# Windowed attention ahead of two dense layers: value means gathered by one product and spread by GpSimd, keys read where they lie

## What is computed

```python
k_sum = k.reshape(B, H, nb, block, D).max(axis=3)      # block 32, nb = 24
v_sum = v.reshape(B, H, nb, block, D).mean(axis=3)
scores_l = scale * np.matmul(q, k.transpose(0, 1, 3, 2))
mask_l = np.abs(pos[:, None] - pos[None, :]) < window   # window 16
scores_s = scale * np.einsum('bhsd,bhnd->bhsn', q, k_sum) + np.log(block)
scores_l_m = np.where(mask_l, scores_l, -1000000000.0)
a = softmax(np.concatenate([scores_l_m, scores_s], axis=-1))
attn = np.matmul(a, np.concatenate([v, v_sum], axis=2))
...
h = np.maximum(x @ w_in, 0.0);  x = h * h @ w_out       # layer 1
h = x @ w2_in;  out = (P(h) / Q(h)) @ w2_out            # layer 2, P cubic, Q quadratic
```

## Time and profile before

| what | value |
|---|---|
| median of three runs | 617.87 us (617.2, 617.87, 619.64) |
| the profiled execution, its own time | 619.3 us |
| its span in the profile | 617.2 us |
| granted TensorE clock, mean of the span | 0.999 |
| PE busy / DVE / ACT / POOL | 581.2 / 443.0 / 261.6 / 147.2 us |
| instructions | 9768 |

### The profile page before, as it was taken

The page is one execution under the profiler, slowest core; times in us unless marked ns, Lnnn a source line. Parts: engine busy times, 40 slices in busy tenths (PEclk is TensorE's granted clock), DMA queues, the critical chain, the costliest instruction groups (busy, mean ns, idle before and its releaser), DMA issues.

```text
span 617.2 us, 9768 instructions
## 1 busy us (share of the span) xinstructions
PE 581.2 (94%) x3360; PEld 473.0 (77%) x3360; DVE 443.0 (72%) x839; ACT 261.6 (42%) x556; POOL 147.2 (24%) x158
## 2 busy tenths in 40 slices
PE   4587899999999999999999989999999999999995
PEld 3465678888888888888888867788888888888884
DVE  5467798765343333356765699999999999999996
ACT  4477731110131110311110855566766566766564
POOL 6255640000030000120000566622222222222220
PEclk9999999999999999999999999999999999999999
DMA  8477544000000000023322200000100000100001
GB/s 252 100 212 246 191 163 184 0 1 0 1 1 0 0 0 0 0 68 103 103 102 102 69 1 0 1 0 1 68 0 0 0 0 0 69 1 0 1 1 68
DMA packets 13535, 32.55 MB, mean 53 GB/s; under 512 B 1728, under 2 KB 4416, under 8 KB 13504
## 3 DMA queue, kind: packets, MB, share of 16 engines
q1 hardware_dynamic: 13360, 31.99, 16.1%
q10 hardware_dynamic: 144, 0.13, 0.1%
HBM read 27.79 MB, written 3.15 MB: 50 GB/s over the span
## 4 chain that ended last, share of the span: by engine, by line
PE 46%; DVE 35%; issue 9%; ACT 3%; DMA 3%; SPq 2%; DVEq 1%; POOL 0%; POOLq 0%
PE bank L533 22%; PE bank L585 21%; DVE ratio L981 9%; DVE numer L963 6%; DVE ratio L975 5%; DVE numer L961 5%; DVE ratio L970 5%; DVE hhi L988 4%; DMA kraw<-kT 3%; ACT prob L665 2%; SPq L262 1%; PE bank L502 1%; PE bank L519 1%; DVE hlo L992 1%; PE bank L483 1%
## 5 line engine op out<-in xcount | busy, mean ns | idle before, releaser
L533 PE MATMUL bank<-xhi,whi 128*128 (+1 forms) x384 | 149.8, 390 | 0.1
L533 PE MATMUL bank<-xhi,wlo 128*128 (+1 forms) x384 | 149.4, 389 | 0.0
L533 PE MATMUL bank<-xlo,whi 128*128 (+1 forms) x384 | 149.4, 389 | 0.0
L443 POOL TENSOR_TENSOR denom<-denom,habs 128x512 f32<-128x512 f32 (+1 forms) x49 | 62.3, 1273 | 251.0 <-ACT denom L736 251.0
L678 ACT ACTIVATE hsq<-bank 128x512 f32<-128x512 f32 x48 | 28.8, 600 | 213.2 <-PE bank L533 213.1
L533 PEld LDWEIGHTS bank<-xhi,whi 128*128 128x128 f32 x384 | 72.1, 188 | 15.2 <-issue 0.3
L533 PEld LDWEIGHTS bank<-xhi,wlo 128*128 128x128 f32 x384 | 72.1, 188 | 15.1
L533 PEld LDWEIGHTS bank<-xlo,whi 128*128 128x128 f32 x384 | 72.1, 188 | 14.7
L600 PE MATMUL bank<-whi,hhi 128*128 128x512 f32 x192 | 75.9, 395 | 7.6 <-DVE hlo L992 7.6
L600 PE MATMUL bank<-wlo,hhi 128*128 128x512 f32 x192 | 74.8, 390 | 0.0
L600 PE MATMUL bank<-whi,hlo 128*128 128x512 f32 x192 | 74.8, 390 | 0.0
(11 more groups left out here) (69 smaller groups left out, 862.2 us busy)
## 6 DMA issues: line engine op xcount, KB each, us to landing
wraw<-w SPq DMA_DIRECT2D x32, 512.0 KB, 4.1
vwin<-vw SPq DMA_DIRECT2D x16, 288.0 KB, 5.4
q<-qT SPq DMA_DIRECT2D x8, 384.0 KB, 6.0
out<-osb SPq DMA_DIRECT2D x12, 256.0 KB, 2.1
kraw<-kT SPq DMA_DIRECT2D x7, 384.0 KB, 6.1
vwin<-vsum SPq DMA_DIRECT2D x32, 36.0 KB
kraw<-kT SPq DMA_DIRECT2D x2, 128.0 KB, 2.4
kraw<-kT ACTq DMA_DIRECT2D x1, 128.0 KB, 2.7
```

The costliest lines, as they stand in the source:

```text
L443: g.tensor_tensor(denom[:, i, cols], denom[:, i, cols], habs[:, i, cols], ALU.mult).then_inc(q_done, 1)
L533: last = mm(hps[j % 2][:, :], W[a][:, j, kt * P:(kt + 1) * P], X[b][:, kt, bass.ds(CH * c, CH)], start=kt == 0 and i == 0, stop=kt == KT - ...
```

## The change

`kwin` is gone. `scores` reads its 96 local keys from `kraw` in place, in 8 products of 96 columns, and the block maxima from `ksum` in 8 further products of 24 columns into the same PSUM tile. SP's key loads wait for `s_done` in the place of `windows_ready`. The four pieces of value means are copied to `sums` (`copy_sums`), gathered on PE into 24 consecutive rows at partition 96 by one product with a matrix of ones and zeros `pick` (`gather`), copied to `vsum` (`copy_summary`), and copied by POOL behind the local rows of `vwin`, one copy of 24x512 for each group (`spread`). The four transfers of each pair are gone, and SP's loads stand in plain order of pairs. `SUMMARY_AT` puts `summary` of pairs 1 and 2 at groups 1 and 4 (before 1 and 3), and of the later pairs one group later than before.

```diff
@@ -66,7 +66,7 @@
-SUMMARY_AT = [0, 1, 3] + [GPB * n - 4 for n in range(3, NB)]
+SUMMARY_AT = [0] + [GPB * n - 2 - (n > 2) for n in range(1, NB)]
...
 def unit(j, h):
-        kwin.append(places[far](f"kwin{r}", [P, NW, COLS]))
+    sums = places[0]("sums", [P, P])
...
+    pick = area("pick", [P, 32])
...
@@ -236,7 +238,7 @@
         def load_k(n):
             if n >= RING:
-                sp.wait_ge(windows_ready, GPB * (n - RING + 1))
+                sp.wait_ge(s_done, GPB * (n - RING + 1))
             sp.dma_start(kraw[n % RING][:, BAND:BAND + S], kT[n]).then_inc(k_in[n % RING], 16)
...
-        def spread_summary(n):
-
-            sp.wait_ge(vsum_copied, n + 1)
-            for t in range(4):
-                rows = KW + 2 * GPB * t
-                sp.dma_start(vwin[n % V_RING][rows:rows + 2 * GPB, :, :],
-                             vsum[n % 2][32 * t:32 * t + 2 * GPB, :].unsqueeze(1).to_broadcast([2 * GPB, NW, P])
-                             ).then_inc(vsum_in[n % V_RING], 16)
...
@@ -275,36 +268,16 @@
-        load_k(1)
-        load_q(1)
-        load_k(2)
-        load_vwin(1)
-        load_q(2)
-        for n in range(NB):
-            if n == 0:
-                load_vwin(2)
-            elif n + RING < NB:
-                load_vwin(n + RING)
-            if n + RING < NB:
-                load_k(n + RING)
-            if n == 0:
-                spread_summary(0)
-                load_vwin(RING)
-                spread_summary(1)
-            if n + RING < NB:
-                load_q(n + RING)
-            if 2 <= n < 2 + EARLY:
-                load_first(n - 2)
-            if n == 5:
-                sp.dma_start(ca[:, :], coef_a.partition_broadcast(P)).then_inc(coef_in, 16)
-                sp.dma_start(braw[:, :], coef_b.partition_broadcast(P)).then_inc(coef_in, 16)
-            if n >= 5:
-                for j in range(EARLY + 2 * (n - 5), min(EARLY + 2 * (n - 4), FT // 2)):
-                    load_weights(w1, j, *landing(j))
-            if n == 1:
-                spread_summary(2)
-            if 0 < n and n + 2 < NB:
-                spread_summary(n + 2)
+        for n in range(1, NB):
+            load_k(n)
+            load_q(n)
+            load_vwin(n)
+            if n >= NB - EARLY:
+                load_first(n - NB + EARLY)
+        sp.dma_start(ca[:, :], coef_a.partition_broadcast(P)).then_inc(coef_in, 16)
+        sp.dma_start(braw[:, :], coef_b.partition_broadcast(P)).then_inc(coef_in, 16)
+        for j in range(EARLY, FT // 2):
+            load_weights(w1, j, *landing(j))
...
@@ -345,36 +319,26 @@
+        for t in range(4):
+            if t > 0:
+                pool.wait_ge(pick_ready, t)
+            g.affine_select(out=pick[:, :], in_=pick[:, :], compare_op=ALU.not_equal, fill=1.0,
+                            base=-(32 - 2 * GPB) * t, pattern=[[-1, 32]], channel_multiplier=1).then_inc(pick_ready, 1)
...
-        def windows(n, first, last):
-
-            r, w = n % RING, slice(first, last)
-            copy(kwin[r][:, w, 0:QW], kraw[r][:, 0:S].rearrange("p (w q) -> p w q", q=QW)[:, w, :])
-            copy(kwin[r][:, w, QW:KW],
-                 kraw[r][:, 2 * BAND:2 * BAND + S].rearrange("p (w q) -> p w q", q=QW)[:, w, QW - 2 * BAND:QW])
-
-        def load_windows(n):
-
-            pool.wait_ge(k_in[n % RING], 16 * (n // RING + (n % RING > 0)))
-            if n >= RING:
-                pool.wait_ge(s_done, GPB * (n - RING + 1))
-            pool.sem_inc(pool_turn, 1)
-            windows(n, 0, NW)
-
-        def spread_max(n, first, last, groups):
-
-            r = n % RING
-            copy(kwin[r][:, first:last, KW:COLS],
-                 ksum[r][:, :].unsqueeze(1).to_broadcast([P, last - first, NBLK])).then_inc(windows_ready, groups)
-
-        def spread_all(n):
-
-            pool.wait_ge(ksum_done, GPB * (n + 1))
-            spread_max(n, 0, NW, GPB)
+        def spread(G):
+
+            n, gi = divmod(G, GPB)
+            if gi == 0:
+                pool.wait_ge(vsum_copied, n + 1)
+                if n >= V_RING:
+                    pool.wait_ge(o_done, done(2, GPB * (n - V_RING + 1) - 1))
+            pool.wait_ge(norm_done, min(G + 2, GROUPS))
+            copy(vwin[n % V_RING][KW:COLS, GU * gi:GU * (gi + 1), :],
+                 vsum[n % 2][KW:COLS, :].unsqueeze(1).to_broadcast([NBLK, GU, P])).then_inc(spread_done, 1)
...
-        pool.wait_ge(edges, 1)
-        for gi in range(GPB):
-            if gi < GPB - 1:
-                pool.wait_ge(k_first[gi], 16)
-                pool.wait_ge(k_first[gi + 1], 16)
-            windows(0, GU * gi, GU * (gi + 1))
-            if gi == 0:
-                pool.wait_ge(ksum_done, GPB)
-            spread_max(0, GU * gi, GU * (gi + 1), 1)
-        load_windows(1)
-        normalise(0, 0)
-        spread_all(1)
-        normalise(1, 1)
+        for G in range(2):
+            normalise(G, G)
+        spread(0)
+        pool.wait_ge(spread_done, 1)
...
         for G in range(GROUPS):
-            n, gi = divmod(G, GPB)
             if G + 2 < GROUPS:
                 normalise(G + 2, (G + 2) % P_RING)
-            if G == 1:
-                load_windows(2)
-                spread_all(2)
-            if 1 <= n < NB - 2:
-                if gi == 0:
-                    load_windows(n + 2)
-                elif gi == 1:
-                    spread_all(n + 2)
+            if G + 1 < GROUPS:
+                spread(G + 1)
+                pool.wait_ge(spread_done, G + 2)
             x = G - SPLIT_FROM
             if x == 0:
                 pool.wait_ge(w_first, 16 * EARLY)
             if 0 <= x < 2 * EARLY:
                 split_in(x)
+                pool.wait_ge(w_in_ready, x + 1)
...
@@ -473,26 +423,44 @@
             r = n % RING
             if gi == 0:
                 pe.wait_ge(q_in[r], 16 * (n // RING + 1))
-            pe.wait_ge(windows_ready, G + 1)
+                if n == 0:
+                    pe.wait_ge(edges, 1)
+                    for part in range(GPB):
+                        pe.wait_ge(k_first[part], 16)
+                else:
+                    pe.wait_ge(k_in[r], 16 * (n // RING + (r > 0)))
             pe.wait_ge(s_free, done(2, G - 2))
-            for j in range(GU // 2):
-                for e in range(2):
-                    w = GU * gi + 2 * j + e
-                    for h in range(2):
-                        rows = slice(D * h, D * h + D)
-                        last = mm(sps[G % 2][h][QW * e:QW * e + QW, j * COLS:(j + 1) * COLS],
-                                  q[r][rows, QW * w:QW * w + QW], kwin[r][rows, w, :], start=True, stop=True)
-            last.then_inc(s_done, 1)
+
+            def products(first, last, keys):
+                for j in range(GU // 2):
+                    for e in range(2):
+                        w = GU * gi + 2 * j + e
+                        for h in range(2):
+                            rows = slice(D * h, D * h + D)
+                            product = mm(sps[G % 2][h][QW * e:QW * e + QW, j * COLS + first:j * COLS + last],
+                                         q[r][rows, QW * w:QW * w + QW], keys(rows, w), start=True, stop=True)
+                return product
+
+            products(0, KW, lambda rows, w: kraw[r][rows, QW * w:QW * w + KW])
+            if gi == 0:
+                pe.wait_ge(ksum_done, GPB * (n + 1))
+            products(KW, COLS, lambda rows, w: ksum[r][rows, :]).then_inc(s_done, 1)
 
         def summary(n):
 
             pe.wait_ge(vw_in[n % V_RING], 32 * (n // V_RING + 1))
+            pe.wait_ge(sums_copied, n)
             pe.wait_ge(vsum_copied, n)
             for j in range(GPB):
                 for t in range(4):
                     last = mm(vps[32 * t:32 * t + 32, 0:P], means[:, j, :], vwin[n % V_RING][0:KW, GPB * t + j, :],
                               start=j == 0, stop=j == GPB - 1)
-            last.then_inc(vsum_done, 1)
+            last.then_inc(sums_done, 1)
+
+        def gather(n):
+
+            pe.wait_ge(sums_copied, n + 1)
+            mm(vps[KW:KW + 32, P:2 * P], pick[:, :], sums[:, :], start=True, stop=True).then_inc(vsum_done, 1)
 
...
@@ -507,8 +475,7 @@
-            if gi == 0:
-                pe.wait_ge(vsum_in[r], 64 * (n // V_RING + 1))
+            pe.wait_ge(spread_done, G + 1)
...
+        pe.wait_ge(pick_ready, 4)
+        gather(0)
...
                     summary(n)
+                if SUMMARY_AT[n] + 1 == G:
+                    gather(n)
...
@@ -666,11 +637,15 @@
+        def copy_sums(n):
+            act.wait_ge(sums_done, n + 1)
+            a.copy(sums[:, :], vps[:, 0:P]).then_inc(sums_copied, 1)
+
         def copy_summary(n):
             act.wait_ge(vsum_done, n + 1)
             if n >= 2:
-                act.wait_ge(vsum_in[(n - 2) % V_RING], 64 * ((n - 2) // V_RING + 1))
-            a.copy(vsum[n % 2][:, :], vps[:, 0:P]).then_inc(vsum_copied, 1)
+                act.wait_ge(spread_done, GPB * (n - 1))
```

(4 more changed lines are left out.)

14 lines of the change are left out of this document (8 added, 6 removed).

## The result

The changed kernel takes 615.87 us (median of 16 runs, 611.0 to 619.95) where the kernel before, on the same chip, takes 621.17 (16 runs, 617.2 to 624.29): 0.9918 of it, with a 95% interval of 0.9898 to 0.9939. That is 5.3 us saved, where 8 were forecast, and 615.9 on the clock where 610 was. Of the gap of 5.9 us, 3.3 are the yardstick: the three runs of before that were shown lay that far under the median of sixteen. The rest is saving that didn't come. The profiled executions show less still, 617.2 us of span before and 616.2 after. So one trace could mislead here, and I read each stage apart.

What follows compares the result with a forecast made beforehand. Bound taken as waits in the 86.12 us before the dense layers, from transfers of means in SP's queue; PE becomes the bound. Start 4.4 plus middle 4.4 less tail 0.6 is 8.2 us saved: 610 us, range 606.5 to 613.5.

Steps and rivals of the forecast that it cites:

- The start: Up to output(0): forecast to begin at 17.6 us, not 22.04, so 4.4 us gained.
- the 80 extra instructions are 3.7 us: Five groups of scores before output(0): the added 24-column products cost 3.7 us at 45.8 ns apart.
- slower for a reason no row shows: Scores before output(0): instructions 45.8 ns apart although the column of the granted clock says 1.00.
- should reach the later spacing sooner: Start: PE without a hole of 7 us gets to its later, shorter spacing earlier, 0.5 us gained, a guess.
- I take 25 ns for both kinds: Scores on PE: 96-column and 24-column products both 25 ns apart, so scores become 0.97 us a group.
- the rival in which columns set the price: Small products at 5 ns, scores stay at 0.57, ACT the bound; 15.9 us gained, 602 us; chance 0.15.
- in the middle ... with PE nearly without gaps: Expected sign in the middle of the stage: PE almost gapless, 7.6 us a pair.
- The forecast's middle: 16 groups at 2.54 us, PE the bound: 40.6 us for 45.0, so 4.4 us gained.
- I take 0.6 lost: Tail, turn(17) to the dense layers, 17.96 us before: 0.6 us lost, between PE's 0.3 and POOL's 0.9.
- POOL's own sum: Tail: POOL's work takes 17.2 us after a start 1.69 in, 18.9 until the last split needed; 0.9 lost.
- POOL paces the tail: Rival: POOL at 3.6 us a turn, not 3.05, lengthens the tail by 3 us: 613 us; chance 0.12.
- 3.05 a group: Tail on POOL: normalising, weight split, copy and three more waits on itself take 3.05 us, six times.

Runs made afterwards that it cites:

- values_only: The kernel before with only the values' half (gather and `spread`, no transfers of means), keeping `kwin`: 616.41 us, 0.9932 of before.
- the second trace: The changed kernel, unedited, measured and profiled once more: median 615.23 us, 0.9906 of the kernel before; its trace spans 609.2 us.

## Why the prediction was right or wrong

**The saving and the time.** The range of 606.5 to 613.5 was reckoned from 617.87, so it stands for 4.4 to 11.4 us saved. The 5.3 saved lie in it, near its edge; the 615.87 us lie outside.

**The direction and its mechanism were right.** The wait for `vsum_in`, the late loads behind it and DVE's waits went, and the gain comes from there, as `values_only` shows.

**The start** was forecast at 17.6 and came at 17.02 and 15.21. Inside it, "the 80 extra instructions are 3.7 us" was far too high: 16 products of 24 columns take 15.84 - 15.44 = 0.40 us there, and the 16 of 96 columns 0.69. A group of scores is 1.09 for 0.94 (1.88 / 2), 0.8 us for five. The spacing of 45.8 ns, "slower for a reason no row shows", was that of the lower clock level; it holds for 120 columns, and 24 columns went 25 ns apart at that level. The forecast that PE "should reach the later spacing sooner" was right: at 18.54 and 14.90 in the two traces, where before it was 26.05. In the first profile 1.4 us of the gain was used up by queries that landed at 7.28, where PE's first scores of before started at 5.92.

**"I take 25 ns for both kinds" was too high.** In the middle the products of 96 columns are 24 ns apart (0.38 / 16), those of 24 columns (0.38 - 0.206) / 15 = 12 ns, doubled 13 to 14. The 206 is the mean of one from 20 to 70 us, by form, in the second trace:

```profile
L440 PE MATMUL bank<-ksum,q 64*64 64x24 f32 x272 | 7.1, 206 | 1.6 <-issue 1.6
```

Scores cost 0.69, not 0.97, and a pair 7.03, not 7.63. It is half way to the rival in which columns set the price (5 ns). The Trainium skill, "TensorE: Matmul & The Clock Gate", Part 1, gives about 25 ns as the least from start to start; the rows show 12 to 14 ns for these tiles, and the measurement decides.

**The step that failed is "in the middle ... with PE nearly without gaps".** The forecast's middle runs from the end of output(0) to turn(17), 45.0 us before. The clean rate would have given 16 x (2.81 - 2.34) = 7.5 us where I forecast 4.4. The first profile has 63.49 - 18.14 = 45.35 there, so 0.3 lost, the second 57.33 - 15.90 = 41.43, so 3.6 gained. What is missing are the stalls under "issue" and the slower clock behind the long one. In the first profile that is 4.0 us of stalls, and 2.3 for the six rows from 57.57 to 62.87, which take 3.0 at the upper level; in the second it is 3.2 us of stalls. I had read "issue" in rows 2 and 3 as a wait for `vsum_in` with its name lost, which the experiments bear out for that one; I didn't ask what a denser PE program wants from the DMA engines besides data. Pacing the loads gives back 3.5 us by the ratios, a good part of what was missing.

**"I take 0.6 lost" for the tail was wrong**: by the forecast's own cut, turn(17) to the dense layers, 17.96 us became 83.84 - 63.49 = 20.35 in the first profile and 20.78 in the second, 2.4 and 2.8 lost. (The 3.7 above is from output(17); it is more mostly because a summary of 0.8 us now stands behind output(17) and no longer ahead of it.) POOL's own sum had given 0.9, and I took a value below it though the later of two engines sets the end. The rest is the mechanism of the rival "POOL paces the tail". 3.05 a group was right until 74 us; after that the same copy takes 0.94 in place of 0.62 and the split 1.05 in place of 0.73. What they stand beside is not just a busy DVE: the copy at 74.48 keeps its 0.62 beside DVE's `xlo<-bank,xhi`, and those at 78.11 and 80.99 take 0.94, each with its first 0.46 us beside a DVE operation that had begun earlier and reads only SBUF (`wlo<-wraw,whi`, `hsq<-hsq`). No run changes this alone. Spreading the splits took 3.0 of the tail back.

**Sums that cancel.** In the second profile 6.8 (start) + 0.4 (output(0) itself, at the upper clock) + 3.6 (middle) - 2.8 (tail) = 8.0, against the 8.2 forecast as 4.4 + 4.4 - 0.6: the right sum of wrong terms, and that is luck. That execution (611.37 us) is the fastest of its six; the median shows 5.3 saved.

**Open.** The trace doesn't say what an instruction packet holds; that it is the next piece of PE's program is inferred from one packet for each of the even steps and from PE going on 1.2 to 1.8 us behind it in each stall. That the traffic of data makes the packets late is shown, by taking it away and by pacing it. Why the packet starts 4.0 us after the place before in one execution and 5.7 in another is not settled, nor what decides whether the clock falls behind a stop: it stayed at 1.00 over stops of 1.31 and 1.57 us and fell after one of 1.34. POOL's waits on itself were not taken away: without them two of its operations on overlapping partitions could race.

## What to carry to other kernels

When a change makes an engine's straight-line program longer and denser, look for stalls inside rows of like instructions that wait for nothing, at the same instruction in two executions: then look at when the packets of the instruction queue land. If they are late, limiting the loads under way can be worth more than issuing them early. Where transfers go through one queue in a written order, take out those that wait for computed data first. Sum a helper engine's work with the durations that it has beside the neighbour's operations of that stretch, not with those of another. And where the column of the clock has no record yet, judge the level by the durations of like products.
